# Attention's products in fewer, longer stretches of TensorE's order: a kernel of linear attention, convolution and two feed-forward layers

## What is computed

```python
# attention: one state of D x D per batch and head, walked over the tokens
for t in range(S):
    cur = np.einsum('bhd,bhe->bhde', u[None] * kt, vt)
    y[:, :, t] = np.einsum('bhd,bhde->bhe', rt, state + cur)
    state = w[None, :, :, None] * state + np.einsum('bhd,bhe->bhde', kt, vt)
# layer one: 384 -> 1024, relu, a gate from a convolution over three tokens, -> 384
h = np.maximum(x @ w_in, 0.0)
gate = 1.0 / (1.0 + np.exp(-conv_out))          # conv_out: conv_w over h at t-1, t, t+1
x = h * gate @ w_out
# layer two: normalised, 384 -> 1536, relu, -> 384, added to x
xn = (x - mu) / np.sqrt(var + 1e-06) * g_ln
out = x + np.maximum(xn @ w_ch1, 0.0) @ w_ch2
```

## Time and profile before

| | before |
|---|---|
| median of three runs (range) | 639.19 us (639.11 to 639.89) |
| the profiled execution, its own time | 639.75 us |
| its span, first to last instruction | 637.5 us |
| TensorE busy | 615.8 us, 97% of the span, 4434 matmuls |
| VectorE, ScalarE, GpSimd busy | 424.8, 260.4, 133.0 us |
| TensorE's granted clock | 1.000 of 2.4 GHz, mean |
| chain that ended last | TensorE 91%, VectorE 4%, issue 1% |

### The profile page before, as it was taken

How to read it: one execution, slowest core, us unless ns; L and a number is a source line. 1 busy time by engine, 2 the same in 40 slices (tenths; PEclk the granted TensorE clock), 3 DMA queues, 4 the chain that set the end, 5 groups by cost and what they waited for, 6 DMA issues and landing times.

```text
span 637.5 us, 10898 instructions
## 1 busy us (share of the span) xinstructions
PE 615.8 (97%) x4434; PEld 558.9 (88%) x4434; DVE 424.8 (67%) x689; ACT 260.4 (41%) x466; POOL 133.0 (21%) x139
## 2 busy tenths in 40 slices
PE   2899999999999999999999999999999999999997
PEld 2787989999998999999999989989999999989996
DVE  7899986798556686555885556865649754376343
ACT  1266644364333264331743423643316534165330
POOL 4741054300432102421003321033010031000200
PEclk9999999999999999999999999999999999999999
DMA  8980230211302311101022023121110100010001
GB/s 216 317 282 30 88 101 16 67 43 32 101 1 67 110 30 61 44 30 52 30 66 69 0 68 108 30 67 39 44 66 7 61 1 1 1 43 1 0 1 42
DMA packets 15200, 38.78 MB, mean 61 GB/s; under 512 B 2096, under 2 KB 8112, under 8 KB 15152
## 3 DMA queue, kind: packets, MB, share of 16 engines
q1 hardware_dynamic: 15152, 38.10, 19.1%
HBM read 33.37 MB, written 4.72 MB: 60 GB/s over the span
## 4 chain that ended last, share of the span: by engine, by line
PE 91%; DVE 4%; issue 1%; DMA 1%; ACT 1%; POOL 1%; SPq 0%; DVEq 0%; POOLq 0%
PE hid L396 14%; PE acc L396 13%; PE hid L397 13%; PE hid L398 13%; PE acc L398 13%; PE acc L397 13%; PE att_ps L410 3%; PE att_ps L450 3%; PE att_ps L445 2%; PE att_ps L424 1%; PE att_ps L457 1%; DMA raw_n<-rk_n 1%; PE acc L544 1%; PE hid L410 0%; DVE w_raw L701 0%
## 5 line engine op out<-in xcount | busy, mean ns | idle before, releaser
L396 PE MATMUL acc<-ring_hi,w_hi 128*128 128x440 f32 (+1 forms) x420 | 153.6, 366 | 0.3 <-DVE ring_lo L790 0.3
L398 PE MATMUL acc<-ring_hi,w_lo 128*128 128x440 f32 (+1 forms) x420 | 151.8, 361 | 0.0
L397 PE MATMUL acc<-ring_lo,w_hi 128*128 128x440 f32 (+1 forms) x420 | 151.4, 360 | 0.0
L623 ACT ACTIVATE ring_hi<-hid 128x440 fp32r<-128x440 f32 (+1 forms) x84 | 45.1, 536 | 178.8 <-PE hid L398 176.4
L827 DVE SCALAR_TENSOR_TENSOR ring_lo<-hid,ring_hi 128x440 fp32r<-128x440 f32 (+1 forms) x84 | 50.8, 611 | 92.9 <-ACT ring_hi L623 92.9
L396 PE MATMUL hid<-x_hi,w_hi 128*128 128x440 f32 (+1 forms) x252 | 94.6, 375 | 0.5 <-DVE ring_lo L827 0.3
L397 PE MATMUL hid<-x_lo,w_hi 128*128 128x440 f32 (+1 forms) x252 | 91.5, 363 | 0.0
L398 PE MATMUL hid<-x_hi,w_lo 128*128 128x440 f32 (+1 forms) x252 | 91.2, 362 | 0.0
L396 PEld LDWEIGHTS acc<-ring_hi,w_hi 128*128 128x128 f32 x420 | 78.9, 188 | 6.4 <-issue 0.6
L398 PEld LDWEIGHTS acc<-ring_hi,w_lo 128*128 128x128 f32 x420 | 78.8, 188 | 5.2
L397 PEld LDWEIGHTS acc<-ring_lo,w_hi 128*128 128x128 f32 x420 | 78.9, 188 | 4.7
(11 more groups left out here) (128 smaller groups left out, 950.6 us busy)
## 6 DMA issues: line engine op xcount, KB each, us to landing
rk<-rk_t SPq DMA_DIRECT2D x22, 448.0 KB, 3.6
raw_n<-rk_n SPq DMA_DIRECT2D x22, 384.0 KB, 3.7
w_raw<-weights SPq DMA_DIRECT2D x10, 768.0 KB, 14.6
v_sb<-v_n SPq DMA_DIRECT2D x22, 192.0 KB, 2.4
out<-x SPq DMA_DIRECT2D x18, 220.0 KB, 2.2
first_rk<-rk_t SPq DMA_DIRECT2D x2, 448.0 KB, 11.3
first_raw_n<-rk_n SPq DMA_DIRECT2D x2, 384.0 KB, 11.5
out<-x SPq DMA_DIRECT2D x3, 218.0 KB, 2.1
```

Source lines behind the costliest of these rows:

```text
L396: mm(ps, lh, rh, start=start, stop=False)
L397: mm(ps, lh, rl, start=False, stop=False)
L398: return mm(ps, ll, rh, start=False, stop=stop)
L623: nc.scalar.activation(ring_hi[:, tile % RING, 0:n], hid[f % 2][:, 0:n], ACT.Relu).then_inc(act_hi, 1)
```

## The change

The five lists for units 1 to 6 are written anew; the engines' work is the same, instruction for instruction. Beside them one wait is added: SyncE's loads of a chunk's values and tokens, which reuse the buffers of the chunk two before, also wait for that chunk's `kv`, since `kv` now stands behind `y` or `xt` in two places. The list is cut here to the lines around the first joined stretch:

```diff
 PE_PLAN = [
...
-    ("mm2", 4), ("scores", 1), ("mm2", 5), ("xt", 0), ("mm2", 6, 7), ("kv", 1), ("y", 1),
-    ("ffn1", 0), ("ffn1", 1), ("xt", 1), ("ffn1", 2), ("ffn2", 0), ("ffn1", 3), ("ffn2", 1), ("total", 0),
-    ("ffn1", 4), ("ffn2", 2), ("scores", 2), ("ffn1", 5), ("ffn2", 3), ("ffn1", 6), ("total", 1), ("ffn2", 4),
...
+    ("y", 0), ("kv", 0), ("mm2", 1), ("mm1", 7), ("mm2", 2), ("xt", 0), ("scores", 1), ("mm2", 3), ("mm2", 4),
+    ("mm2", 5), ("mm2", 6, 7), ("kv", 1), ("y", 1), ("scores", 2), ("xt", 1), ("ffn1", 0), ("ffn1", 1),
...
                 sp.wait_ge(pe_y, loaded_over(m) + 1)
                 load_t(m)
                 sp.wait_ge(pe_xt, loaded_over(m) + 1)
+                sp.wait_ge(pe_kv, states_made(loaded_over(m)))
                 load_v(m)
                 load_n(m)
```

More of the change, by code:

```diff
@@ L98 @@
 ACT_PLAN = [
[L99 to L107, removed]
+    ("relu", 0), ("relu", 1), ("sig", 0), ("relu", 2), ("hi", 0), ("sig", 1), ("relu", 3), ("sig", 2), ("relu", 4),
+    ("hi", 1), ("hi", 2), ("relu", 5), ("sig", 3), ("relu", 6), ("sig", 4), ("sig", 5), ("hi", 3), ("relu", 7),
+    ("hi", 4), ("hi", 5), ("sig", 6), ("sig", 7), ("hi", 6), ("xh", 0), ("hi", 7), ("x2_hi", 0), ("x2", 0),
+    ("x2_hi", 1), ("x2_hi", 2), ("xh", 1), ("x2", 1), ("x2", 2), ("fhi", 0), ("fhi", 1), ("fhi", 2), ("sum_hi", 0),
+    ("fhi", 3), ("square", 0), ("fhi", 4), ("square", 1), ("square", 2), ("fhi", 5), ("sum_hi", 1), ("fhi", 6),
+    ("fhi", 7), ("root",), ("fhi", 8), ("xh", 2), ("fhi", 9), ("fhi", 10), ("fhi", 11), ("xh", 3), ("table",)]
 DVE_FIRST = [
@@ L125 @@
 DVE_PLAN = [
[L126 to L136, removed]
@@ L137 @@
-    ("scale", 3), ("x_low", 3),
-    ("scaled", 0), ("scaled", 1), ("result", 0), ("scaled", 2), ("result", 1), ("result", 2)]
+    ("conv", 0), ("scale", 0), ("gated", 0), ("conv", 1), ("masked", 0, 0), ("conv", 2), ("gated", 1), ("low", 0),
+    ("gated", 2), ("conv", 3), ("low", 1), ("masked", 0, 1), ("low", 2), ("conv", 4), ("gated", 3), ("conv", 5),
+    ("gated", 4), ("x_sum", 0), ("state", 0), ("low", 3), ("conv", 6), ("gated", 5), ("low", 4), ("conv", 7),
+    ("low", 5), ("gated", 6), ("gated", 7), ("low", 6), ("dots", 0), ("low", 7), ("masked", 1, 0), ("scale", 1),
@@ new lines @@
+    ("x_low", 0), ("x2_low", 0), ("masked", 1, 1), ("state", 1), ("x_sum", 1), ("x2_low", 1), ("dots", 1),
+    ("x2_low", 2), ("flow", 0), ("x_low", 1), ("flow", 1), ("flow", 2), ("masked", 2, 0), ("sum_low", 0),
+    ("off_mean", 0), ("flow", 3), ("flow", 4), ("off_mean", 1), ("off_mean", 2), ("masked", 2, 1), ("dots", 2),
+    ("sum_low", 1), ("flow", 5), ("flow", 6), ("variance",), ("flow", 7), ("state", 2), ("scale", 2), ("newton",),
+    ("x_sum", 2), ("flow", 8), ("flow", 9), ("masked", 3, 0), ("scale", 3), ("masked", 3, 1), ("flow", 10),
@@ L139 @@
+    ("x_low", 2), ("x_sum", 3), ("flow", 11), ("dots", 3), ("x_low", 3), ("scaled", 0), ("result", 0),
+    ("scaled", 1), ("result", 1), ("state", 3), ("scaled", 2), ("result", 2)]
 POOL_FIRST = [
@@ L143 @@
 POOL_PLAN = [
-    ("pad",), ("ruk", 0), ("kd", 0), ("cv", 0), ("sums", 0), ("ruk", 1), ("kd", 1), ("cv", 1), ("sums", 1),
-    ("ruk", 2), ("kd", 2), ("cv", 2), ("ruk", 3), ("kd", 3), ("cv", 3)]
+    ("ruk", 0), ("kd", 0), ("ruk", 1), ("cv", 0), ("cv", 1), ("sums", 0), ("ruk", 2), ("sums", 1), ("cv", 2),
+    ("kd", 1), ("kd", 2), ("ruk", 3), ("kd", 3), ("cv", 3), ("pad",)]
 SP_FIRST = [
@@ L152 @@
     ("loads", 8), ("results", 0), ("results", 1), ("results", 2)]
-SP_PLAN = [("loads", 0), ("loads", 1), ("loads", 2), ("loads", 3), ("results", 0), ("results", 1), ("results", 2)]
+SP_PLAN = [
+    ("loads", 0), ("loads", 1), ("loads", 2), ("loads", 3), ("results", 0), ("results", 1), ("results", 2)]
 LATER = {"scale": 1, "ruk": 1, "dots": 1, "cv": 1, "kd": 1, "loads": 2}
```

## The result

The changed kernel takes 634.08 us, the median of four runs (633.84 to 634.28), beside 639.38 for the kernel before on the same chip: a ratio of 0.9916 [0.9899, 0.9933]. The prediction was 634.5 (633.0 to 637.0). The profiled execution took 634.28 us against 639.75, its span 632.0 against 637.5.

What follows compares the result with a forecast made beforehand. TensorE, busy 97% of the span, was taken as the path. Terms summed to -5.0 us, -4.7 with +0.3 for new waits: 635.0 from the profiled 639.75, set to 634.5 because that run lay 0.56 above the median; range 633.0 to 637.0.

Steps and rivals of the forecast that it cites:

- The long stretch: TensorE, five units: `kv` 1, `y` 1, scores 2, `xt` 1 joined gain 0.45 us each, -2.2 in all.
- The 20.3 us that I gave for the five stretches apart: Sign of being wrong: TensorE's five long stretches sum near 20.3 us, what their parts cost apart.
- Joins worth nothing: Rival, 15%: each change of shape on TensorE costs as much as returning to wide products; -3.2 us, so 636.0.
- transposes then scores: TensorE, `xt` 0 + scores 1, five times: 1.61 us joined against 1.62 apart, so gain 0.
- `y` 3, then `xt` 3 + `kv` 3: TensorE, unit 1 alone: `kv` leaves the values and stands behind transposes, costing +0.3 us.
- scores then transposes: TensorE, scores 3 + `xt` 2, twice: joining gains 0.06 us each, -0.1 in all.
- Scores 3: TensorE's 0.89 us idle until `scale` was done goes, with state 2 and `scale` 2 ahead of `newton`: -1.8 us.
- Unit 6: Tile 4 of `mm1` no longer waits for relu 2, now first in ScalarE's list: -0.9 us; two shorter waits left.
- New waits: Misses of less than a tenth of a microsecond in each of five long stretches: +0.3 us in all.
- What I feared of `masked` (1, 1): Rival, 10%: VectorE, held by `masked` (1, 1) and others, makes state 1 late and the long stretch wait; 639.2.
- GpSimd's collisions: Rival, 7%: GpSimd's `ruk` 1 slows VectorE's `low` 7 and `scale` 1, holding `mm2` 1.7 us in five units; 642.8.
- My last rival, that more comes out: Rival, 8%: unit 6's two shorter waits go, new waits cost nothing, values to scores gain 0.49; near 633.2 us.

Runs made afterwards that it cites:

- the cut kernel: Changed kernel with its long stretch cut in three (scores 2, `xt` 1 between `ffn1` tiles) and ScalarE's and VectorE's lists mended to fit: 635.69 us, 0.9937.
- the unmended cut: Changed kernel with scores 2 and `xt` 1 put between the tiles of `ffn1`, other engines' lists left as they were: 658.00 us, 1.0290.
- the late state: Changed kernel with VectorE's `x_sum` 1 moved ahead of `state` 1: 648.24 us, 1.0125.

## Why the prediction came out

- **The bound.** TensorE's list was the path and stayed it: its last start moved by 5.3 us and the run by 5.3 to 5.5. Adding up prices along one engine's list worked because that engine has next to no idle time.
- **The long stretch.** Predicted 0.45 a time, measured 0.40 or 0.41 (4.07 to 3.66, 3.41 to 3.01 in unit 2). I chose near the end that values to `kv` gave (1.61). It measured 163.82 - 162.12 = 1.70, and the cut kernel shows the same 1.70 from the values to a wide product (162.18 to 163.88), which waits for no state. So the scores weren't held by the state: of what was seen behind the values, `kv` alone is cheaper (1.61 in the earlier trace rows, 1.63 in the changed kernel). The 20.3 us that I gave for the five stretches apart were wrong for unit 2, whose values lack the state's products (3.41): they cost 19.7, without harm to a difference.
- **Joins worth nothing**, my first rival, fell in its own terms: it gave 3.2 us for the sum, and the mended cut shows that three stretches joined into one save 0.24 us over and above the ready transposes. Its example holds, though: transposes then scores cost 1.61 joined, as the earlier trace rows had it. The Trainium skill's TensorEngine Tiling (Array Packing), section Tiling Modes, says that a change of mode drains the engine. This trace agrees in direction once the changes are counted right. In the prediction I counted the transposes as a shape of their own, but the rows give 128\*128 for them and for the wide products alike. So the long stretch (the values' products counted as one shape) has one change of shape fewer than its parts, and saves 0.24 us; transposes then scores have none fewer, and save nothing; `y` 3, then `xt` 3 + `kv` 3 have one more than before, and cost 0.32 more (2.95 against 2.63). It isn't the whole of it: scores then transposes have none fewer either and save 0.06, and no run changed the shape by itself.
- **Scores 3.** -1.8 predicted, -1.9 measured, and alone in a kernel of its own -1.8 (0.9976).
- **Unit 6** is the term that was mis-sized: -0.9 predicted, -1.5 measured. `relu` 2 gave 1.0; the 0.5 beyond it is the wait ahead of the last `mm2`, which I had seen and left as it was. With the changed lists in unit 6 alone it goes, with `relu` 2 alone it stays, so it hangs on another entry of the lists. Its row in the trace of the kernel before was there to be followed back, to VectorE's `low`:

```profile
585.35 0.43 PE L396 MATMUL acc<-ring_hi,w_hi 128*128 128x436 f32 x1 [0.28 <-DVE ring_lo L790]
```

  TensorE's own list is the likeliest cause: between the end of `mm1` 7 and this `mm2` it had 27 wide products, `mm2` 3 to 5, and now has 36, `mm2` 2 to 5, which is 1.8 us more for `low`. Before, `low` ended at 585.20, 0.5 us behind the last of the 27 starts (584.70); now it ends at 579.69, and TensorE gets there at 580.14. This is read from the traces; that entry wasn't tried by itself.
- **New waits.** +0.3 predicted, 0 measured. The slack for the state was 0.07 us where I had worked out 0.1. What I feared of `masked` (1, 1) didn't come: VectorE was idle for 1.10 us ahead of the state, and half of that could be filled at no cost.
- **GpSimd's collisions** came, smaller than priced, and were covered. In unit 2 VectorE's timeline has `low` 7 and `scale` 1 longer than alone (0.62 and 1.22):

```profile
244.01 0.97 DVE L787 TENSOR_TENSOR ring_lo<-conv_sb,ring_hi 128x440 fp32r<-128x440 f32 x1
...
245.51 1.43 DVE L710 TENSOR_TENSOR rk<-rk,powrk 112x1024 f32<-112x1024 f32 x1
```

  beside GpSimd's `ruk` 1:

```profile
243.44 1.08 POOL L879 TENSOR_TENSOR raw_n<-raw_n 128x384 f32<-128x384 f32 x1 [24.46 <-DMA raw_n<-rk_n]
244.59 1.27 POOL L881 TENSOR_TENSOR raw_n<-raw_n,u_b 128x384 f32<-128x384 f32 x1
```

  That is 0.35 + 0.21 us, a third of the 1.7 that the rival took from the convolution step, and `mm2` never waited.
- **The sum and some luck.** The two errors of size point the same way: +0.3 for waits that weren't there, and 0.6 too little for unit 6. The trace became 5.5 us shorter (637.5 to 632.0) where I had 4.7. That the median came within 0.4 us (634.08 for 634.5) is in part luck: before, the profiled execution lay 0.56 above the median I started from, now it lies 0.20 above its own. My last rival, that more comes out, came half true: the new waits cost nothing and one of unit 6's two shorter waits went, but values to scores did not gain their 0.49.

## What to carry to other kernels

Where one engine's list is the path, give every run of odd work in it a price, from the last regular start ahead to the second one behind, and every change of order becomes a sum over such prices. Of the gain here less than a quarter (1.15 of 5.3 us) came from joining as such; more, some 3.3 us, came from three moves on other engines, which took away TensorE's waits at three places and shortened the end. An order of the busiest engine is only as good as the lists beside it. Before moving work there, ask of each result that becomes later what stands behind its reader in that reader's queue: other engines' entries left where they stood made 22 of the 24 us that one kernel here lost (658.00 against 635.69 with them moved), and a single entry on the wrong side of `state` 1 cost another kernel 14.

## What the runs showed of the hardware that was not expected

Short idle times cost TensorE its clock in some places and not in others. With the late state, TensorE was idle for 1.93 us ahead of the scores in units 1 and 3, and wide starts behind it stood 0.37 us apart instead of 0.20, the 1.2 GHz level. In unit 5 it was the same; in unit 4 the idle time was alike to the hundredth, and the pitch stayed 0.20:

```profile
434.12 1.16 PE L407 MATMUL att_ps<-rk 48*128 48x128 f32 x16 [1.93 <-issue]
...
435.52 0.44 PE L393 MATMUL hid<-x_hi,w_hi 128*128 128x440 f32 x1
435.80 0.36 PE L394 MATMUL hid<-x_lo,w_hi 128*128 128x440 f32 x1
```

The windows around four of the five places give the granted clock (the last but two of the columns):

```profile
160.00:172.00 12.00, 10.07 (x109) 9.13 (x108) 4.54 (x9) 3.87 (x8) 2.72 (x4) 0.86 0.26 83
...
340.00:352.00 12.00, 10.07 (x93) 9.25 (x88) 5.03 (x10) 2.42 (x5) 5.13 (x5) 0.86 0.28 89
431.00:443.00 12.00, 10.07 (x92) 9.39 (x89) 6.23 (x13) 3.43 (x7) 5.12 (x5) 1.00 0.28 89
517.00:529.00 12.00, 10.07 (x95) 9.30 (x92) 5.03 (x10) 2.46 (x6) 3.08 (x3) 0.86 0.01 1
```

(In unit 2 TensorE was idle for 1.3 us only.) The kernel with the unmended cut was idle for 2.5 us in each of the five units, and has 0.86 in units 1, 3 and 5 and 1.00 in units 2 and 4 too. What a fall costs is read from the start of the long stretch to the start of the next one (`kv` 2 + `y` 2), against the changed kernel: 31.73 for 29.73 us in unit 4, but 33.27 for 29.74 in unit 3, and as much in units 1 and 5. So a later start of 2.0 us stayed 2.0 in unit 4 and became 3.5 or 3.6 in the three others: 1.5 or 1.6 us a fall. What tells unit 4 from unit 3 is open.
